# An even diagonal as VectorE products and TensorE sums, K's first update in the layer before, and a changed order of steps

## What is computed

```python
for t in range(S):                      # 8 heads of 48, per batch
    state = alpha[t][:, None] * state + outer(k[t], v[t])
    y[t] = q[t] @ state
x = y as (B, 768, 384)
xk = mu_k * x + (1 - mu_k) * x_prev;  xr likewise with mu_r
x = sigmoid(xr @ w_r) * (relu(xk @ w_k) ** 2 @ w_v)          # 384 -> 1024 -> 384
u = x + (x.T @ U @ V).T                                      # mixing over tokens, rank 32
out = u + relu(u @ w_ch1) @ w_ch2                            # 384 -> 1536 -> 384
```

## Time and profile before

| | us |
|---|---|
| median of 3 runs (lowest to highest) | 758.43 (756.23 to 759.75) |
| profiled execution | 757.66 |
| its span | 755.9 |
| busy: TensorE, its weight loads, VectorE, ACT, GpSimd | 718.0, 678.3, 428.5, 252.8, 60.8 |

### The profile page before, as it was taken

The page is one execution under the profiler, slowest core; times in us unless marked ns, Lnnn a source line. Parts: engine busy times, 40 slices in busy tenths (PEclk is TensorE's granted clock), DMA queues, the critical chain, the costliest instruction groups (busy, mean ns, idle before and its releaser), DMA issues.

```text
span 755.9 us, 22449 instructions
## 1 busy us (share of the span) xinstructions
PE 718.0 (95%) x10120; PEld 678.3 (90%) x10120; DVE 428.5 (57%) x751; ACT 252.8 (33%) x498; POOL 60.8 (8%) x123
## 2 busy tenths in 40 slices
PE   4777989999999999999999999999999999989998
PEld 4677979889999999979999999979999999969998
DVE  4788869772696338662496427754387525341312
ACT  1344545233424153233333234232442324321211
POOL 3401102000010001100021001100011000000000
PEclk9999989999999999999999999999999999999999
DMA  8655320003300051000500024000610000000000
GB/s 225 189 168 204 95 84 2 2 2 96 107 3 2 2 153 48 3 2 17 180 7 3 1 79 124 2 3 2 167 34 3 2 9 33 1 0 1 30 3 32
DMA packets 17647, 39.97 MB, mean 53 GB/s; under 512 B 2800, under 2 KB 8560, under 8 KB 17552
## 3 DMA queue, kind: packets, MB, share of 16 engines
q1 hardware_dynamic: 17456, 38.48, 17.1%
q10 hardware_dynamic: 96, 0.07, 0.0%
HBM read 32.64 MB, written 4.72 MB: 49 GB/s over the span
## 4 chain that ended last, share of the span: by engine, by line
PE 88%; DVE 5%; issue 2%; ACT 2%; DMA 1%; SPq 1%; POOL 0%; DVEq 0%; ACTq 0%
PE acc L615 13%; PE acc L616 12%; PE acc L617 12%; PE hps L615 12%; PE hps L616 11%; PE hps L617 11%; PE aps L438 5%; PE hps L703 2%; PE aps L570 2%; PE aps L589 2%; PE aps L449 1%; PE aps L547 1%; DVE QK L1065 1%; DMA QK<-in_q 1%; PE aps L525 1%
## 5 line engine op out<-in xcount | busy, mean ns | idle before, releaser
L1256 DVE SCALAR_TENSOR_TENSOR hid_l<-hps,hid_h 128x384 fp32r<-128x384 f32 x96 | 53.5, 557 | 195.1 <-ACT hid_h L951 195.0
L951 ACT ACTIVATE hid_h<-hps 128x384 fp32r<-128x384 f32 x96 | 47.2, 492 | 203.9 <-PE hps L617 195.7
L615 PE MATMUL hps<-in_h,w_h 128*128 128x384 f32 x288 | 99.0, 344 | 0.7 <-DVE in_l L1236 0.6
L616 PE MATMUL hps<-in_l,w_h 128*128 128x384 f32 x288 | 96.8, 336 | 0.0
L617 PE MATMUL hps<-in_h,w_l 128*128 128x384 f32 x288 | 96.8, 336 | 0.0
L616 PE MATMUL acc<-w_l,hid_h 128*128 128x384 f32 x288 | 96.6, 336 | 0.0
L615 PE MATMUL acc<-w_h,hid_h 128*128 128x384 f32 x288 | 96.6, 335 | 0.0
L617 PE MATMUL acc<-w_h,hid_l 128*128 128x384 f32 x288 | 96.3, 335 | 0.0
L1065 DVE TENSOR_TENSOR QK<-QK,T 112x768 f32<-112x768 f32 x80 | 77.1, 973 | 12.9 <-PE aps L438 11.6
L919 ACT ACTIVATE tmp<-hps 128x384 f32<-128x384 f32 x64 | 31.5, 493 | 148.9 <-PE hps L617 148.0
L1374 POOL TENSOR_TENSOR T<-T 112x384 f32<-112x384 f32 (+4 forms) x80 | 42.3, 532 | 473.9 <-DVE QK L1074 310.7
(11 more groups left out here) (123 smaller groups left out, 1251.2 us busy)
## 6 DMA issues: line engine op xcount, KB each, us to landing
QK<-in_k SPq DMA_DIRECT2D x16, 336.0 KB, 4.1
QK<-in_q SPq DMA_DIRECT2D x16, 336.0 KB, 4.7
T<-in_alpha SPq DMA_DIRECT2D x16, 336.0 KB, 7.2
vt<-in_v SPq DMA_DIRECT2D x16, 288.0 KB, 7.6
raw<-in_w_ch SPq DMA_DIRECT2D x6, 768.0 KB, 6.6
out<-x SPq DMA_DIRECT2D x24, 192.0 KB, 2.0
QK<-in_q_odd SPq DMA_DIRECT2D x16, 168.0 KB, 6.1
raw_k<-in_w_k SPq DMA_DIRECT2D x3, 512.0 KB, 4.9
```

Of the source, the lines that this page charges most:

```text
L615: pe.matmul(o, a[0], b[0], start=first, stop=False)
L616: pe.matmul(o, a[0], b[1], start=False, stop=False)
L951: nc.scalar.activation(hid[0][:, f % 2, :], hps[f % 2][:, 0:HT], ACT.Relu).then_inc(s_rel2, 1)
L1256: nc.vector.scalar_tensor_tensor(out=hid[1][:, f % 2, :], in0=hps[f % 2][:, 0:HT], scalar=0.0, in1=hid[0][:, f % 2, :].bitcast(F32), op0=A ...
```

## The change

- **Even diagonal, units 3 to 7.** VectorE multiplies even q by even k elementwise (`even_qk`, 112 x 768, in a free part of `Pm`); TensorE sums over the 48 features with four products whose weights are ones, one for each half z of the blocks and each group e. The empty step behind level 0 is gone for these units.
- **K's first update** of these units and the even product (`begin`) stand in VectorE's `mlp` behind hid_l of f = 10. In `levels` VectorE then starts with the first Q product, waits for the sums and the moves, keeps the diagonal, and does the second Q product.
- **SyncE**: q and k of the next unit are asked for ahead of the moves, alpha, q_odd and v behind them; `y_split` lies in `Pm` from unit 2 on, so alpha doesn't wait for the moves.
- **Opening**: one level-0 step less of unit 1 ahead of the first mix, three low parts ahead of y instead of two, FIRST and LOWS changed, and in `channel_mix(0, 0)` ACT computes both squares.
- **Unit products** (`fill`): products of the identity with itself into a free bank, 10 + 8 + 10 in `channel_mix(0, 0)`, 12 in `channel_mix(0, 1)`, 6 + 5 in the last token mixing. Nobody reads them.
- **Lists**: BESIDE1 of units 4 and 6 has `low_two` still at f = 1 and the fourth level a part later; BESIDE3 is one step shorter. BESIDE0 is unchanged, so the steps of odd units come a part earlier.

```diff
+        even_qk = Pm[:].rearrange("p y e t -> p (y e t)")[0:HR, 0:S]
...
+        def y_split(n):
+            if n > 1:
+                return Pm[:].rearrange("p y e t -> p (y e t)")[0:HR, S:S + HT]
+            return unit(n).y_split()
...
-            def load_unit(n):
+            def load_qk(n):
...
+            def load_rest(n):
+                b, half = n // 2, n % 2
+                if n == 2:
+                    sp.wait_ge(s_split, 32 * KT)
+                for g in range(2):
+                    sp.dma_start(part(T[0:HR], g), alpha[b, half, g]).then_inc(s_lda[g], 16)
                 for g in range(2):
                     sp.dma_start(odd(units[2].q_odd(), g), q_odd[b, half, g]).then_inc(s_ldo[g], 16)
-                sp.wait_ge(s_split, 32 * KT * (n if n > 2 else 1))
-                for g in range(2):
-                    sp.dma_start(part(T[0:HR], g), alpha[b, half, g]).then_inc(s_lda[g], 16)
+                if n > 2:
+                    for g in range(2):
+                        load_v(n, g)
...
             for n in range(2, 2 * NB):
+                if n + 1 < 2 * NB:
+                    load_qk(n + 1)
                 move_split(n)
                 if n + 1 < 2 * NB:
-                    load_unit(n + 1)
-                    for g in range(2):
-                        load_v(n + 1, g)
+                    load_rest(n + 1)
                 store((n - 2) // 2, n % 2)
...
+            def even_sums(n):
+                pe.wait_ge(s_eqk, n - 2)
+                pe.wait_ge(s_x, n)
+                for z in range(2):
+                    for e in range(2):
+                        rows = slice(e * HS, e * HS + D)
+                        terms = even_qk[rows, :].rearrange("p (y z i) -> p z y i", z=2, i=W2)[:, z]
+                        mm = pe.matmul(bank(n, 0, e)[z * HS:(z + 1) * HS, 0:2 * NC * W2].rearrange(
+                            "p (y i) -> p y i", i=W2), ones[rows, :], terms, start=True, stop=True)
+                        if z == 1:
+                            mm.then_inc(s_dg[e], 1)
...
+                if n > 2:
+                    even_sums(n)
...
+                if n < 3:
+                    yield
...
-                turn_u(b, 1, 1, lambda: None if b == NB - 1 else kept(pe, 2 * b + 3, ML, 1))
+                turn_u(b, 1, 1, lambda: None if b == NB - 1 else pe.wait_ge(s_kt, kx_count(2 * b + 4)))
...
+            def fill(to, count):
+                for _ in range(count):
+                    pe.matmul(to[:, 0:P], ident[:], ident[:], start=True, stop=True)
...
+                if first:
+                    fill(acc[2], 10)
                 step(plan[0])
+                if s == 1:
+                    fill(hps[1], 12)
...
+                    if first and f == 1:
+                        fill(hps[1], 10)
                     step(plan[1 + f])
+                    if first and f == 0:
+                        kept(pe, 1, 0, 1)
+                        fill(hps[1], 8)
...
+                if b == NB - 1:
+                    fill(aps[1], 6)
...
+                if b == NB - 1:
+                    fill(aps[1], 5)
...
+                    if opens(s):
+                        ge(act, s_out, f - 1)
+                        nc.scalar.activation(hid[0][:, f % 2, :], tmp[:, 0, :], ACT.Square).then_inc(s_hh, 1)
...
+            def update_k(n, g):
+                u = unit(n)
+                loaded(dve, n, s_lda, g)
+                k_even, t_odd = left(part(u.K(), g), 0), right(part(u.T[0:HR], g), 0)
+                nc.vector.tensor_tensor(k_even, k_even, t_odd, ALU.mult).then_inc(s_Ke[g], 1)
+            def begin(n):
+                u = unit(n)
+                for g in range(2):
+                    loaded(dve, n, s_ldq, g)
+                    loaded(dve, n, s_ldk, g)
+                dve.wait_ge(s_own, 6 * n)
+                nc.vector.tensor_tensor(even_qk, left(u.Q(), 0), left(u.K(), 0), ALU.mult).then_inc(s_eqk, 1)
+                dve.wait_ge(s_eqk, n - 2)
+                for g in range(2):
+                    update_k(n, g)
...
+                if n > 2:
+                    double(n, 0, 0)
                     for g in range(2):
+                        dve.wait_ge(s_dg[g], n + 1)
+                    dve.wait_ge(s_split, 32 * KT * n)
+                    for e in range(2):
+                        keep(n, 0, e)
+                    double(n, 0, 1)
+                    yield
...
-                low(NR)
-                low(NR + 1)
+                for n in LOW_ORDER[:3]:
+                    low(n)
                 keep_odd(0)
-                next(other)
                 next(other)
...
+                    if after is not None and f == F2 - 2:
+                        begin(after)
...
-            for n in (NR + NK, NR + NK + 1):
-                low(n)
+            next(steps)
...
-                mlp(b, 0, step, BESIDE2, lambda: mix(b + 1, 0, 0), late=late_lows(LATE2 if b == 0 else {}))
+                mlp(b, 0, step, BESIDE2, lambda: mix(b + 1, 0, 0), late=late_lows(LATE2 if b == 0 else {}, 2 * b + 3))
...
-                mlp(b, 1, step, BESIDE3, lambda: mix(b + 1, 1, 0))
+                mlp(b, 1, step, BESIDE3, lambda: mix(b + 1, 1, 0),
+                    late=late_lows({}, 2 * b + 4 if b < NB - 2 else None))
...
-FIRST = [1, 1, 1, 1, 1, 1, 1, 3, 2, 0]
-BESIDE1 = [1, 1, 1, 1, 1, 1, 0, 1, 0, 0]
+FIRST = [0, 2, 1, 1, 1, 1, 1, 3, 2, 0]
+BESIDE1_FIRST = [1, 1, 1, 1, 1, 1, 0, 1, 0, 0]
+BESIDE1 = [1, 0, 1, 1, 1, 0, 1, 1, 0, 0]
 BESIDE_T = [1, 1, 1]
 BESIDE2 = [0, 1, 1, 0, 1, 1, 0, 0, 0, 0, 0, 0]
 BESIDE0 = [1, 1, 1, 1, 1, 1, 1, 0, 1, 0]
-BESIDE3 = [0, 1, 1, 1, 1, 0, 1, 1, 0, 0, 0, 0]
+BESIDE3 = [0, 1, 1, 1, 0, 1, 1, 0, 0, 0, 0, 0]
 HIGHS = [0, 0, 0, 1, 1, 1, 1, 1, 1, 2, 0, 0, 0, 0]
-LOWS = [0, 0, 0, 0, 1, 1, 1, 1, 2, 1, 0, 0, 1, 0]
+LOWS = [0, 0, 0, 1, 1, 1, 1, 1, 2, 1, 0, 0, 1, 0]
 LAST = [0, 1, 0, 2, 2, 1, 0, 0, 0, 0, 0, 0, 0, 0]
 LATE = {4: slice(0, 2), 6: slice(2, 4)}
```

More of the change, by code:

```diff
@@ L100, in build @@
         ident = sb("ident", [P, P])
+        ones = sb("ones", [P, HS])
         level_mask = sb("level_mask", [P, MW], U8)
@@ L779, in _ @@
                 step = stepper(steps)
-                channel_mix(b, 1, step, BESIDE1, first_g(b))
+                channel_mix(b, 1, step, BESIDE1 if b > 0 else BESIDE1_FIRST, first_g(b))
                 token_mix(b, step, BESIDE_T)
@@ L800, in levels @@
             def levels(n):
-                for _ in range(LV + 1):
+                for _ in range(LV + 1 if n < 3 else LV):
                     yield
@@ L816, in keep_split @@
                 rows = slice(e * HS, e * HS + D)
-                return nc.scalar.copy(unit(n).y_split()[rows, :], y_all[rows, 0:HT])
+                return nc.scalar.copy(y_split(n)[rows, :], y_all[rows, 0:HT])
             def keep_rest(n, e, crossed):
@@ L1007, in _ @@
                 step = stepper(steps)
-                channel_mix(b, 1, step, BESIDE1)
+                channel_mix(b, 1, step, BESIDE1 if b > 0 else BESIDE1_FIRST)
                 token_mix(b, step, BESIDE_T)
@@ L1065, in double @@
                 nc.vector.tensor_tensor(qk, qk, t, ALU.mult).then_inc(s_qk[g], 1)
+            def update_k(n, g):
[11 more added lines that the diff above has]
+                dve.wait_ge(s_eqk, n - 2)
+                for g in range(2):
+                    update_k(n, g)
             def levels(n):
                 u = unit(n)
-                for g in range(2):
-                    dve.wait_ge(s_dg[g], n + 1)
-                    loaded(dve, n, s_lda, g)
-                    k_even, t_odd = left(part(u.K(), g), 0), right(part(u.T[0:HR], g), 0)
-                    nc.vector.tensor_tensor(k_even, k_even, t_odd, ALU.mult).then_inc(s_Ke[g], 1)
-                    if opens(n):
-                        double(n, 0, g)
-                for e in range(2):
-                    keep(n, 0, e)
-                yield
-                if not opens(n):
-                    for g in range(2):
-                        double(n, 0, g)
-                yield
+                if n > 2:
+                    double(n, 0, 0)
+                    for g in range(2):
+                        dve.wait_ge(s_dg[g], n + 1)
+                    dve.wait_ge(s_split, 32 * KT * n)
+                    for e in range(2):
+                        keep(n, 0, e)
+                    double(n, 0, 1)
+                    yield
+                else:
+                    for g in range(2):
+                        dve.wait_ge(s_dg[g], n + 1)
+                        update_k(n, g)
+                        if opens(n):
+                            double(n, 0, g)
+                    for e in range(2):
+                        keep(n, 0, e)
+                    yield
+                    if not opens(n):
+                        for g in range(2):
+                            double(n, 0, g)
+                    yield
                 for g in range(2):
@@ L1134, in keep_odd @@
                 dve.wait_ge(s_y, 3 * n + 2)
```

(15 more changed lines are left out.)

37 lines of the change are left out of this document (18 added, 19 removed).

## The result

| kernel | us, median (lowest to highest) | profiled span |
|---|---|---|
| before | 757.9 (754.86 to 759.75), 20 executions | 755.9 |
| after | 760.07 (757.77 to 762.14), 20 executions | 758.3 |

The ratio of after to before is 1.0031, 95% interval 1.0020 to 1.0041: slower, by less than the 0.5% that I took as the bound. The forecast was 759.5. Each program has one profile, and its executions spread over 2 to 8 us, so a single trace says where time goes and the medians say how much.

A forecast was written before the change was run, and what follows sets the result against it. TensorE was taken as the bound (88% of the chain), with little VectorE slack where work is added. Opening -2.0, end +0.2, odd units +3.9, even units -0.2 sum to +1.9 on 757.7; forecast 759.5 us, range 752.0 to 764.5.

The forecast's parts named there:

- Even sums: Even diagonal, units 3 to 7: four sums take 0.8 us instead of 1.54, so -0.7 us of TensorE per unit.
- Serial quadrants: Rival for the even sums: quadrants run one after another, 2.8 us, total 767 us; chance 0.05.
- program order: Rival for the even sums: five steps of 0.354, 1.8 us, total 761.5 us; chance 0.07.
- `begin` at the layer's end: Second layer's last parts: VectorE's added work delays the last hid_l and TensorE's addition, +0.6 us per unit.
- Odd units: Start of units 3, 5, 7: TensorE waits 0.9 us before `low_two`, 0.5 before the first addition; +3.9 us with layer ends.
- Per unit: Steady state, units 3 to 7: +1.3 us for each odd unit, -0.1 for each even one.
- Side relief: Odd units' start: GpSimd's T products no longer overlap VectorE's Q products (pair 2.31 us, 1.82 without); nothing charged beside hid_l.
- Loads ahead of moves: SyncE's queue: four issues of some 0.45 us and 1.3 MB ahead of six moves cost nothing, either way.
- Opening: First layer: new order and fills bring TensorE's first addition to 67.0 us from 68.98, -2.0 us; bounds -0.7 and +2.3.
- Unit products: Fills in opening and end: 0.24 us each, up to twice that; ten from 46 us at 1.2 GHz end at 50.8.
- End: Last token mixing: eleven fills, 2.6 us, in two waits of 1.2, +0.2 us; clock already full there.
- The rival of no new waits: Steady state: VectorE's added work fits beside TensorE, five times 0.7 us gained, total 752.4 us; chance 0.24.

The follow-up runs named there:

- e6: Kernel after, with each unit's four sums of the even diagonal issued twice; 761.84 us, ratio to before 1.0044.
- e2: Kernel after, with `begin` two parts earlier, behind hid_l of f = 8 instead of f = 10; 757.74 us, ratio to before 1.0003.
- e1: Kernel after, with list BESIDE0 altered so `low_two` of units 3, 5 and 7 comes at f = 1 again; 754.54 us, ratio to before 0.9955.
- e3: Kernel after, with the edits of both e1 and e2; 752.07 us, ratio to before 0.9914.
- e8: Kernel after, with ACT's squares undone (VectorE computes hid_h) and y's moves ahead of all loads again; 760.16 us, ratio to before 1.0023.
- e7: Kernel of e3, with alpha of units 3 to 7 also asked for ahead of y's moves; 752.90 us, ratio to before 0.9920.
- e5: Kernel before, with the opening's edits alone: new order, ACT's squares, the opening's unit products; 757.69 us, ratio to before 0.9991.
- e4: Kernel after, with all 51 unit products left out; 760.19 us, ratio to before 1.0025.
- e9: Kernel of e3, with all 51 unit products left out; 752.79 us, ratio to before 0.9944.
- e12: Kernel of e3, with only the first ten unit products kept; 753.47 us, ratio to before 0.9951.

## Why the prediction was right, and where it was not

The total was right (759.5 for 760.07), and the likeliest case is the one that came, with its waits where it put them. From span to span the forecast was +1.9 us and +2.4 were measured. That the absolute time is 0.6 us off is in part luck, as 757.7, on which the sum stands, is a single execution and happens to lie 0.2 from the median of 20.

- **Even sums**: 0.8 us forecast, 0.81 measured from first to next. Taking the price from `low_two`, which alternates over the same quadrants, and not from the one wide fp32 product, was right. Serial quadrants (2.8) and program order (1.8) are out (e6).
- **`begin` at the layer's end**: +0.6 forecast, 0.53 measured, at the five places named, and gone when `begin` moves (e2).
- **Odd units**: the forecast had TensorE at `low_two` at 206.5 and VectorE ready at 207.4. Everything stands 0.94 us earlier in after, as unit 3 starts earlier (199.82 for 200.76). With that added back, TensorE is free at 205.43 + 0.94 = 206.4 and starts at 206.54 + 0.94 = 207.5: a wait of 1.1 for 0.9. The addition's wait is 0.54 for 0.5. Shown by e1, which takes both away, and by e6, whose extra pass disappears in the first.
- **Per unit**: odd +1.3 forecast, +1.54 and +1.48 measured; even -0.1 forecast, -0.35 and -0.37 measured. The steady state comes to +3.75 against +3.7, because two small errors cancel. With the waits gone (e3) an even distance is 0.99 us shorter than before and an odd one up to 0.82 (84.61 to 83.79), where the sums alone give 0.73. No run explains the surplus of about 0.26 in even units.
- **Side relief**: GpSimd's T products moved from beside Q's pair, 2.31 us for two, to beside hid_l. Q's two products now take 0.95 and 0.94, and the updates their usual 1.03 for two. Nothing charged, nothing lost.
- **Loads ahead of moves**: 0, right (e8), but with less to spare than the prediction had. It counted the issues (1.8 us; in after they take 2.9) and not the transfers, by which the moves land 1.9 us later too. In after ACT starts without a wait at 276.37; two more loads bring it (e7).
- **Opening**: -2.0 forecast, -1.5 in the profile, -1.8 to +0.4 by e5. Two steps of this term failed, and they cancel in part. The r products ran at full clock from the first at 49.55, not from 52 us on, and ten unit products took 4.2 us and not 4.8; so the first addition came at 66.11 and not at 67.0, 2.87 us ahead of before. And the sum took the gain there as the gain at the end. Behind it, about 0.85 us went at the place in TensorE's program (1.17 for 0.46, where 0.03 and 0.17 are usual), and 0.36 at the addition behind ACT's squares (0.97 from start to start for 0.61), which the prediction had let vanish in a later wait. Unit 2 starts 1.46 earlier, of which 0.53 was there already when unit 1's level 0 began.
- **Unit products**: 0.24 us each forecast, 0.23 at full clock (eight in 1.81). Their price was right; that they bring the clock forward to the r products was right in 8 of the 10 profiles that have the first ten; that this is worth anything at the end is not borne out (e4, e9). The prediction took the full clock as something that comes once; in e2 and e7 it came earlier and was lost again.
- **End**: +0.2 forecast, +0.1 measured. That the clock is full there already holds for before, e4 and e9; without unit products it fell to half there in e5 and e12, for 1.2 and 2.5 us.
- **The rival of no new waits** (752.4) didn't come in this change. It is nearly the kernel that e3 makes of it, at 752.07. What stood against it was two numbers in the order of work. That the totals agree to 0.3 us is luck in part: the rival took -2.0 for the opening, where -1.5 or less came, and -0.7 for each unit, where e3 has -0.99 in the even ones.

## What to carry to other kernels

When a step or a wait is taken out of a hand-written order, count every list behind it again: what follows moves up one place, and an engine that was ready just in time is then late. Put added work where the helping engine's trace has its longest idle time (2.57 us between hid_l of f = 8 and of f = 9), not where the work is just in time (1.07 us between f = 10 and f = 11); then look whether its loads have landed there. A gain in an opening isn't a term of the sum until it has been followed past the next places where TensorE waits.

## What the runs showed of the hardware

- Four fp32 products of 384 columns in four quadrants, eight records, cost 0.64 us back to back; one such record in a single place costs 0.354.
- A product of the identity with itself (128 columns, fp32) costs 0.23 us at 2.4 GHz and 0.42 at 1.2.
- The clock row can't be trusted in the first 55 us: the table by stretches gives 1.00 for 40 to 50 us in e4, whose r products there stand 0.32 us apart, and 0.53 for the same stretch in after. Seven of the 14 traces give 1.00 there while level 0 of unit 1 runs at half clock. Distances between starts are the safer reading.
- A 24 KB transfer lands 1.9 us after its issue where it stands ahead of the loads, 3.8 behind four loads of 336 KB and 5.7 behind six (medians of 36 or 45).
- TensorE halts at one fixed record of its program, for about a us where it gets there 1.3 to 1.5 us after a 16 KB packet of the instruction queue has started, and for 0.1 to 0.3 where it takes 1.9 to 2.3. The packet ends 1.2 to 1.5 us before TensorE goes on, in all 14 traces.
- Two waits of TensorE of 1.7 and 1.6 us, start to start, in the last token mixing cost it the full clock in two of five profiles (e5, e12) and not in the other three. Unit products in these waits kept it in nine of nine.
